# The first pair's normalisation in fewer sums, with a Newton root, and a changed order on GpSimd

## The chip, the cores and the metric

The kernel runs on one core of one Trainium2 chip. The metric is the device time of one execution in microseconds (us). Five engines run their own instruction streams and meet through semaphores: TensorE (PE in the rows; PEld is its weight load), VectorE (DVE), ScalarE (ACT), GpSimd (POOL) and SyncE (SP, which here only issues DMAs).

## The reference

Windowed attention, then two feed-forward layers on its output (2304 tokens of 512 values):

```python
scores = scale * q @ k.T                      # 4 x 8 heads, 576 tokens, 64 values a head
mask = (rel >= 0) & (rel < 64)                # each query sees the 64 keys up to its own
attn = exp(scores - max) / (sum + 1e-9)
x = (attn @ v), heads joined                  # 2304 x 512
rms = sqrt(mean(x * x, axis=-1) + 1e-6)
xn = x / rms * rms_g
y = (silu(xn @ w_gate) * (xn @ w_val)) @ w_out     # 512 -> 1536 -> 512
out = relu(y @ w_in) ** 2 @ w_down                 # 512 -> 2048 -> 512
```

## The kernel before, in words

Everything is written out by hand: five streams of instructions, one for each engine, in an order that the code fixes, and semaphores between them. No scheduler moves anything.

**Attention** (the first 80 us or so). The 144 query blocks of two heads each are taken in 18 groups of 8 blocks. For group g:

- PE (`slot(g)`) makes the scores of group g, then the product with v of group g-3, then transposes the probabilities of group g-2. Two score buffers alternate.
- DVE merges the two halves of each block's scores (L1468, COPY_PREDICATED), takes the negative maximum (L1475), inverts the row sums of group g-1 (L1480), and writes the masked transpose of group g-2 from PSUM into `probsT` (L1488).
- POOL adds 1e-9 to the row sums of group g-1 (L628), multiplies the negative maxima of group g by the scale (L632, `peak`), and multiplies the probabilities of group g-1 by the inverted sums (L635).
- ACT makes the exponentials of group g with the scaled maximum as bias (L1159), and copies finished attention output into `acts`.

Between these, work for what follows is placed at chosen groups: the split of the first two units' weights in a high and a low part (`high1_plain`, `low1_plain`, `high2_plain`, `low2_plain` on POOL), and the **first pair's normalisation**. A pair is 768 tokens (two halves of 384), and there are three. Its squares are made on POOL and ACT, PE sums them over the 512 values by products with a column of ones (`first_sums`, L817), DVE scales the sum (`mean_square`, L1420), ACT takes the root (`root`, L1119), DVE inverts it (`inverse`, L1425), POOL makes diagonals of the result (`diagonals`, L591), PE spreads them over all partitions (`spread_half`, L825), and DVE multiplies (`normalise`, L1428). ACT then rounds and DVE subtracts, which gives the two halves of a split operand (L1145, and `x_low`, L1460).

**Feed-forward layers** (the rest). PE multiplies split operands in three matmuls each (L844 to L846). The up projections run in units `u`, each of seven products p1 to p7 of six matmuls (a Strassen form). Unit u has POOL sum weights (`weight_sum`, L572 to L584) and multiply results (`h_a`, `h_b`, L672 and L683), DVE write three sums `ga`, `va`, `vb` (L1650, L1658, L1670) and low parts (`low1`, `low2`). The second and third pair's normalisation is made inside the units of the run before: `mean_square` in the unit with s == 8, `root` and `inverse` after it, `diagonals` on POOL at s == 9. PE holds these waits that the prediction speaks of:

```python
def p7(u, r):
    x_ready(u, r, "T3")
    if u > S0[r]:
        pe.wait_ge(c21_done, steps_done(u - 1))   # set by va of the unit before

if g == 18:
    pe.wait_ge(x_split, split_count(0, "B21"))    # set by x_low(0, "B21")
```

Of the kernel before, what the change touches and what calls it, by code (L numbers as in the profile page):

```python
# [29 lines left out]
BF16 = mybir.dt.bfloat16  # L30
ALU = mybir.AluOpType
# [3 lines left out]
P = 128  # L35
# [29 lines left out]
WARM = 6  # L65

# [90 lines left out]
def build(nc, qT, kT, v_rows, w_gate, w_val, w_out, gains, w_in, w_down, outT):  # L157
    with ExitStack() as ctx:
# [45 lines left out]
        rms = sb("rms", [P, TB], F32)  # L204
        assert top[0] <= nc.sbuf_usable_end, (top[0], nc.sbuf_usable_end)
# [4 lines left out]
        squares = [[sb(f"sq{n}_{k}", [P, PW], F32, at + k * PW * 4) for k in range(KT)]  # L210
                   for n, at in enumerate((hs_at, h_at + C1 * PW * 4))]
# [59 lines left out]
        sq_pool = sem("sq_pool")  # L271
        sq_done, sq_sum, ms_mm, ms_done = sem("sq_done"), sem("sq_sum"), sem("ms_mm"), sem("ms_done")
        rms_done, rinv_done, diag_done = sem("rms_done"), sem("rinv_done"), sem("diag_done")
# [134 lines left out]
        def _(sp):  # L408
# [128 lines left out]
        def _(pool):  # L537
# [48 lines left out]

            def diagonals(q):

                pool.wait_ge(rinv_done, q + 1)
                pool.wait_ge(ms_mm, q + 1)  # L590
                nc.gpsimd.tensor_tensor(diag[min(q, 1)][:].rearrange("p (n c) -> p n c", n=TB),  # L591
                                        ident[:].unsqueeze(1).broadcast_to([P, TB, P]),
                                        rms[:].unsqueeze(2).broadcast_to([P, TB, P]), ALU.mult).then_inc(diag_done, 1)
# [25 lines left out]
            def square_half(k, c):  # L619
                of = half_cols(0, k, c)  # L620
                nc.gpsimd.tensor_tensor(squares[0][k][:, c * NT:(c + 1) * NT], of, of, ALU.mult).then_inc(sq_pool, 1)

            for g in range(TAIL):
                n = g - N_LAG
                if 0 <= n < GROUPS:
                    total = sums[:, n % PR, :]
                    pool.wait_ge(exp_done, n + 1)
                    nc.gpsimd.tensor_scalar(total, total, 1e-9, None, ALU.add).then_inc(summed, 1)  # L628
                if g < GROUPS:
                    peak = neg_max[:, g % PR, :]  # L630
                    pool.wait_ge(maxed, g + 1)
                    nc.gpsimd.tensor_scalar(peak, peak, SCALE, None, ALU.mult).then_inc(biased, 1)  # L632
                if 0 <= n < GROUPS:
# [3 lines left out]
                if g == 5:  # L637
                    high1_plain(0)
                if g == 6:
                    low1_plain(0)  # L640
                if g == 7:
                    high2_plain(0)
                    low2_plain(0)
                if g in (8, 9):
                    pool.wait_ge(o_out, O_DONE[A_GROUP + 1])
                    for k in (2 * (g - 8), 2 * (g - 8) + 1):
                        square_half(k, 0)
                if g == 10:
                    high1_plain(1)
                    high2_plain(1)  # L650
                if g == 11:
                    pool.wait_ge(o_out, O_DONE[B_GROUP + 1])
                    square_half(0, 1)
                    square_half(1, 1)
                if g == 13:
                    diagonals(0)
                if g == 14:
                    low1_plain(1)
                if g == 15:
                    low2_plain(1)  # L660
# [69 lines left out]
        def _(pe):  # L730
# [82 lines left out]
            def first_sums(c, ps):  # L813

                for n in range(c * TB // 2, (c + 1) * TB // 2):
                    for k in range(KT):
                        mm = pe.matmul(ps[:, n:n + 1], squares[0][k][:, n * P:(n + 1) * P], ones[:, 0:1],  # L817
                                       start=k == 0, stop=k == KT - 1)
                if c == 1:
                    mm.then_inc(ms_mm, 1)  # L820
# [7 lines left out]
            def spread(q, banks):  # L828

                pe.wait_ge(diag_done, q + 1)  # L830
                for n in range(TB):
                    mm = spread_part(q, banks[n * P // NT], n)
                mm.then_inc(rb_mm, 1)

            def spread_half(c, ps):

                pe.wait_ge(diag_done, 1)
# [24 lines left out]
            for g in range(TAIL):  # L862
                slot(g)
                if g == 10:
# [221 lines left out]
        def _(act):  # L1086
# [22 lines left out]
            def square_half(k, c):  # L1109
                cols = slice(c * NT, (c + 1) * NT)  # L1110
                nc.scalar.activation(squares[0][k][:, cols], half_cols(0, k, c), ACT.Square).then_inc(sq_done, 1)
# [4 lines left out]
            def root(q):  # L1116

                act.wait_ge(ms_done, q + 1)
                nc.scalar.activation(rms[:], rms[:], ACT.Sqrt).then_inc(rms_done, 1)  # L1119
# [27 lines left out]
            for g in range(TAIL):  # L1147
# [15 lines left out]
                if g == B_GROUP + O_LAG:  # L1163
                    act.wait_ge(o_out, O_DONE[B_GROUP + 1])
                    square_half(2, 1)
                    square_half(3, 1)
                if g == 12:
                    root(0)
# [116 lines left out]
            for r in range(RUNS):  # L1285
                X, Y, Z = u_banks(r)[0:2], u_banks(r)[2], u_banks(r)[3]
                for u in range(S0[r], U0[r + 1]):
# [30 lines left out]
                    if r + 1 < PAIRS:  # L1318
# [8 lines left out]
                        if s == 8:  # L1327
                            root(r + 1)
# [67 lines left out]
        def _(dve):  # L1396
# [25 lines left out]
            def inverse(q):  # L1422

                dve.wait_ge(rms_done, q + 1)
                nc.vector.reciprocal(rms[:], rms[:]).then_inc(rinv_done, 1)  # L1425
# [37 lines left out]
            for g in range(TAIL):  # L1463
# [29 lines left out]
                if g == 12:  # L1493
                    mean_square(0, bank[5])
                if g == 13:
                    inverse(0)
# [55 lines left out]
            def square_sum(q, k):  # L1552
                dve.wait_ge(sq_done, 2 + KT * (q - 1) + k + 1)
# [73 lines left out]
            for r in range(RUNS):  # L1627
                X, Y, Z = u_banks(r)[0:2], u_banks(r)[2], u_banks(r)[3]
                for u in range(S0[r], U0[r + 1]):
# [14 lines left out]
                    if s == 9 and r + 1 < PAIRS:  # L1644
                        inverse(r + 1)
# [167 lines left out]
```

## Time and profile before

| | |
|---|---|
| median of 3 runs | 878.12 us (876.03 to 879.7) |
| the profiled execution | 876.42 us, its span 874.7 us |
| busy | PE 98%, DVE 68%, ACT 55%, POOL 53% of the span |
| granted TensorE clock | 0.998 of full speed in the mean |

The span is the time from the first to the last instruction of the profiled execution; what lies around it is 1.7 us. Busy shares are means over the whole span. Times in rows are us from the start of the span; "[x <-ENGINE tile]" is how long the engine stood idle before the row and what ended it.

### The profile page before, as it was taken

The numbers are of one execution on the slowest core, as the hardware profiler recorded it, in microseconds if no ns is written. First come the engines' busy times: TensorE is split into PE (matmuls) and PEld (weight loads), VectorE is DVE, ScalarE is ACT, GpSimd is POOL, SyncE is SP. The second block draws the span as 40 slices with busy tenths as digits, with TensorE's granted clock in tenths as the row PEclk, the third lists the DMA queues.
The fourth block names the chain that finished last, engine by engine and source line by source line (L and its number), as shares of the span: only waits on it lengthen the run. The fifth ranks groups of instructions, "written<-read, shape, count | busy, mean of one in ns | idle before, by whom it ended". The sixth has DMA issues, their size and how long they took to land.

```text
span 874.7 us, 16801 instructions
## 1 busy us (share of the span) xinstructions
PE 854.7 (98%) x6388; PEld 841.5 (96%) x6388; DVE 591.4 (68%) x728; ACT 478.8 (55%) x1005; POOL 466.0 (53%) x473
## 2 busy tenths in 40 slices
PE   7798999999999999999999999999999999999998
PEld 5687999999999999999999999999999999999998
DVE  4758675558567548755557767687577787577982
ACT  5887665545565645455555455454555454555451
POOL 3756398683589765388857368400187400386100
PEclk9999999999999999999999999999999999999999
DMA  8863122222222212222212222256632166522687
GB/s 281 263 220 87 49 73 73 61 61 61 84 73 70 70 55 61 79 73 73 73 55 64 81 67 73 56 158 228 218 87 72 56 218 184 176 73 97 182 256 237
DMA packets 107871, 100.18 MB, mean 115 GB/s; under 512 B 6928, under 2 KB 85776, under 8 KB 107792
## 3 DMA queue, kind: packets, MB, share of 16 engines
q1 hardware_dynamic: 92544, 84.14, 32.3%
q10 hardware_dynamic: 15248, 14.98, 4.9%
q8 instruction: 51, 0.84, 0.4%
q14 instruction: 28, 0.23, 0.1%
HBM read 79.69 MB, written 19.40 MB: 113 GB/s over the span
## 4 chain that ended last, share of the span: by engine, by line
PE 90%; DVE 5%; issue 2%; ACT 1%; DMA 1%; POOL 1%; DVEq 0%; ACTq 0%; POOLq 0%
PE banks L844 29%; PE banks L845 28%; PE banks L846 28%; PE banks L803 1%; PE banks L745 1%; DVE probsT L1488 1%; ACT probs L1159 1%; PE banks L817 1%; DMA w_kept<-stash 1%; PE banks L777 1%; DVE acts L1428 0%; DVE banks L1468 0%; DVE d_lo L1574 0%; DVE xc_lo L1460 0%; PE banks L753 0%
## 5 line engine op out<-in xcount | busy, mean ns | idle before, releaser
L844 PE MATMUL banks<-xc_hi,w_hi 128*128 128x384 f32 x844 | 282.6, 335 | 0.2 <-DVE xc_lo L1460 0.2
L846 PE MATMUL banks<-xc_hi,w_lo 128*128 128x384 f32 x844 | 281.9, 334 | 0.0
L845 PE MATMUL banks<-xc_lo,w_hi 128*128 128x384 f32 x844 | 281.9, 334 | 0.0
L844 PE MATMUL banks<-hs_hi,d_hi 128*128 128x384 f32 x544 | 182.4, 335 | 2.3 <-DVE d_lo L1574 2.2
L846 PE MATMUL banks<-hs_hi,d_lo 128*128 128x384 f32 x544 | 181.8, 334 | 0.0
L845 PE MATMUL banks<-hs_lo,d_hi 128*128 128x384 f32 x544 | 181.7, 334 | 0.0
L844 PEld LDWEIGHTS banks<-xc_hi,w_hi 128*128 128x128 f32 x844 | 158.4, 188 | 0.6 <-DVE xc_lo L1460 0.4
L845 PEld LDWEIGHTS banks<-xc_lo,w_hi 128*128 128x128 f32 x844 | 158.4, 188 | 0.0
L846 PEld LDWEIGHTS banks<-xc_hi,w_lo 128*128 128x128 f32 x844 | 158.4, 188 | 0.0
L1405 DVE TENSOR_TENSOR w_lo<-w_raw,w_hi 128x1024 fp32r<-128x1024 f32 x58 | 77.1, 1329 | 81.8 <-ACT w_hi L1090 81.8
L572 POOL TENSOR_TENSOR w_raw<-w_raw 128x256 f32<-128x256 f32 x58 | 60.8, 1047 | 134.0 <-DMA w_raw<-in_w_in 113.6
L1566 DVE TENSOR_TENSOR hs_lo<-h,hs_hi 128x768 fp32r<-128x768 f32 x68 | 68.6, 1009 | 80.5 <-ACT hs_hi L1090 80.2
L1090 ACT ACTIVATE hs_hi<-h 128x768 fp32r<-128x768 f32 x68 | 57.4, 844 | 104.4 <-PE banks L846 99.9
L1090 ACT ACTIVATE w_hi<-w_raw 128x1024 fp32r<-128x1024 f32 x116 | 109.3, 942 | 0.0
L844 PEld LDWEIGHTS banks<-hs_hi,d_hi 128*128 128x128 f32 x544 | 102.1, 188 | 4.0 <-DVE d_lo L1574 2.9
L845 PEld LDWEIGHTS banks<-hs_lo,d_hi 128*128 128x128 f32 x544 | 102.1, 188 | 0.0
L846 PEld LDWEIGHTS banks<-hs_hi,d_lo 128*128 128x128 f32 x544 | 102.1, 188 | 0.0
L690 POOL TENSOR_TENSOR d_lo<-d_raw,d_hi 128x512 fp32r<-128x512 f32 x36 | 54.9, 1524 | 68.2 <-ACT d_hi L1090 68.2
L683 POOL TENSOR_TENSOR h<-sbb,vb 128x384 f32<-128x384 f32 x34 | 55.7, 1638 | 26.1 <-ACT sbb L1199 25.9
L1414 DVE TENSOR_TENSOR w_lo<-w_raw,w_hi 128x768 fp32r<-128x768 f32 x58 | 69.4, 1197 | 0.0
L1205 ACT ACTIVATE sa<-ga 128x384 f32<-128x384 f32 x58 | 30.5, 526 | 67.3 <-DVE ga L1650 67.1
L1090 ACT ACTIVATE c_t<-banks 128x384 f32<-128x384 f32 x58 | 28.5, 492 | 65.3 <-PE banks L846 65.3
(114 smaller groups left out, 1342.5 us busy)
## 6 DMA issues: line engine op xcount, KB each, us to landing
w_kept<-stash SPq DMA_DIRECT2D x56, 256.0 KB, 3.1
w_raw<-in_w_gate SPq DMA_DIRECT2D x36, 256.0 KB, 2.9
w_raw<-in_w_val SPq DMA_DIRECT2D x72, 128.0 KB, 2.8
d_raw<-in_w_out SPq DMA_DIRECT2D x36, 256.0 KB, 2.6
d_raw<-in_w_down SPq DMA_DIRECT2D x32, 256.0 KB, 3.0
v_sb<-in_v_rows SPq DMA_DIRECT2D x16, 384.0 KB, 5.0
w_raw<-in_w_in SPq DMA_DIRECT2D x24, 256.0 KB, 2.7
w_raw<-in_w_in SPq DMA_DIRECT2D x48, 128.0 KB, 2.6
```

What stands on the lines that cost most here:

```text
L572: nc.gpsimd.tensor_tensor(raw_part(u, RAW_S3), raw_part(u, RAW_A11), raw_part(u, RAW_A21), ALU.subtract).then_inc(s_add, 1)
L683: nc.gpsimd.tensor_tensor(h_half(n, 1), sbuf_b[:], vb[:], ALU.mult).then_inc(hb_done, 1)
L690: nc.gpsimd.tensor_tensor(d_lo[m % 2][:], d_raw[m % 2][:], d_hi[m % 2][:].bitcast(F32), ALU.subtract).then_inc(dlo_done, 1)
L745: mm = pe.matmul(to, q_sb[par][r, b * WIN:(b + 1) * WIN], both, start=b > 0, stop=True)
L844: pe.matmul(ps, w_h, v_h, start=first, stop=False, skip_group_check=joined)
L845: pe.matmul(ps, w_h, v_l, start=False, stop=False, skip_group_check=joined)
L846: return pe.matmul(ps, w_l, v_h, start=False, stop=last, skip_group_check=joined)
L1090: nc.scalar.activation(to, of, ACT.Copy).then_inc(done, 1)
L1205: nc.scalar.activation(sa[:], ga[:], ACT.Silu if first_layer(r) else ACT.Relu).then_inc(act_a_done, 1)
L1405: nc.vector.tensor_tensor(w_lo[u % 2][:, to], w_raw[u % 2][:, of], w_hi[u % 2][:, to].bitcast(F32), ALU.subtract).then_inc(lo1_done, 1)
L1414: nc.vector.tensor_tensor(w_lo[u % 2][:, to], w_raw[u % 2][:, of], w_hi[u % 2][:, to].bitcast(F32), ALU.subtract).then_inc(lo2_done, 1)
L1566: nc.vector.tensor_tensor(hs_lo[m % 2][:], h_chunk(r, chunk_of(r, m - M0[r])), hs_hi[m % 2][:].bitcast(F32), ALU.subtract).then_inc(hlo_do ...
```

## The change

Its parts, in the order of the diff:

- The first and second `load_w` are issued at i = 4 and 6 of SP's load loop, not 1 and 3; the first two `load_d` at 10 and 11, not 9 and 10.
- The first pair's squares go two blocks at a time (`square_two`, one POOL instruction for 128x768 where there were two of 128x384), the two halves of the 512 values are added (on POOL for the first half of the tokens, on DVE for the second), and `first_sums` takes 12 matmuls for each half of the tokens where it took 24. It stands after slots 11 and 13, not 10 and 12.
- `root` on ACT and `inverse` on DVE are gone. `inverse_root` on DVE makes the inverse root of all three pairs from an integer seed and two Newton steps: seven instructions on 128x6 values, each waiting for the one before.
- The first pair's diagonals are made in two halves, at groups 13 and 14.
- POOL scales the maximum of group g before it adds to the sums of group g-1, where the order was the other way.
- The split of the first weights moves on POOL from groups 5 to 7, 10, 14 and 15 to groups 12 and 14 to 18.

```diff
-                if i in (1, 3):
-                    load_w((i - 1) // 2)
-                if i in (9, 10):
-                    load_d(i - 9)
+                if i in (4, 6):
+                    load_w((i - 4) // 2)
+                if i in (10, 11):
+                    load_d(i - 10)
...
+            def first_diagonals(c):
+                n = TB // 2
+                pool.wait_ge(rinv_done, STEPS)
...
             for g in range(TAIL):
                 n = g - N_LAG
-                if 0 <= n < GROUPS:
-                    total = sums[:, n % PR, :]
-                    pool.wait_ge(exp_done, n + 1)
-                    nc.gpsimd.tensor_scalar(total, total, 1e-9, None, ALU.add).then_inc(summed, 1)
                 if g < GROUPS:
                     peak = neg_max[:, g % PR, :]
                     pool.wait_ge(maxed, g + 1)
                     nc.gpsimd.tensor_scalar(peak, peak, SCALE, None, ALU.mult).then_inc(biased, 1)
                 if 0 <= n < GROUPS:
+                    total = sums[:, n % PR, :]
+                    pool.wait_ge(exp_done, n + 1)
+                    nc.gpsimd.tensor_scalar(total, total, 1e-9, None, ALU.add).then_inc(summed, 1)
...
+                if g in (8, 9):
+                    pool.wait_ge(o_out, O_DONE[A_GROUP + 1])
+                    square_two(g - 8, 0)
+                if g == 10:
+                    pool.wait_ge(sq_pool, 2)
+                    nc.gpsimd.tensor_tensor(sq_all[:, 0:2, 0:NT], sq_all[:, 0:2, 0:NT], sq_all[:, 2:4, 0:NT],
+                                            ALU.add).then_inc(sq_added, 1)
+                if g == 11:
+                    pool.wait_ge(o_out, O_DONE[B_GROUP + 1])
+                    square_two(0, 1)
+                if g == 12:
                     high1_plain(0)
-                if g == 6:
+                if g == 13:
+                    first_diagonals(0)
+                if g == 14:
+                    first_diagonals(1)
                     low1_plain(0)
...
-                if g == 14:
+                if g == 17:
                     low1_plain(1)
...
-                if g == 10:
+                if g == 11:
                     pe.wait_ge(consts, CONSTS)
-                    pe.wait_ge(sq_pool, KT)
+                    pe.wait_ge(sq_added, 1)
                     first_sums(0, bank[5])
-                if g == 12:
-                    pe.wait_ge(sq_pool, KT + 2)
-                    pe.wait_ge(sq_done, 2)
+                if g == 13:
+                    pe.wait_ge(sq_added, 2)
                     first_sums(1, bank[5])
...
+            def inverse_root(q):
+                done = STEPS * q
+                dve.wait_ge(ms_done, q + 1)
+                nc.vector.tensor_scalar(guess[:].bitcast(I32), rms[:].bitcast(I32), -0.5, ROOT_SEED, ALU.mult,
+                                        ALU.add).then_inc(rinv_done, 1)
+                for n, (by, plus) in enumerate(ROOT_STEPS):
+                    dve.wait_ge(rinv_done, done + 1 + 3 * n)
+                    nc.vector.tensor_tensor(resid[:], guess[:], guess[:], ALU.mult).then_inc(rinv_done, 1)
+                    dve.wait_ge(rinv_done, done + 2 + 3 * n)
+                    nc.vector.scalar_tensor_tensor(out=resid[:], in0=resid[:], scalar=by, in1=rms[:], op0=ALU.mult,
+                                                   op1=ALU.mult).then_inc(rinv_done, 1)
+                    dve.wait_ge(rinv_done, done + 3 + 3 * n)
+                    nc.vector.scalar_tensor_tensor(out=guess[:], in0=resid[:], scalar=plus, in1=guess[:], op0=ALU.add,
+                                                   op1=ALU.mult).then_inc(rinv_done, 1)
...
                 if g == 12:
+                    dve.wait_ge(sq_pool, 3)
+                    dve.wait_ge(sq_done, 1)
+                    nc.vector.tensor_tensor(sq_all[:, 0:2, NT:PW], sq_all[:, 0:2, NT:PW], sq_all[:, 2:4, NT:PW],
+                                            ALU.add).then_inc(sq_added, 1)
+                if g == 13:
                     mean_square(0, bank[5])
-                if g == 13:
-                    inverse(0)
+                    inverse_root(0)
...
                     if s == 9 and r + 1 < PAIRS:
-                        inverse(r + 1)
+                        inverse_root(r + 1)
```

How POOL's stream stands at groups 16 and 17, the last two with a maximum. Before:

```order
L628 TENSOR_SCALAR sums<-sums 128x8
L632 TENSOR_SCALAR neg_max<-neg_max 128x8
L635 TENSOR_TENSOR probs_114<-probs_114,sums 128x512
L628 TENSOR_SCALAR sums<-sums 128x8
L632 TENSOR_SCALAR neg_max<-neg_max 128x8
L635 TENSOR_TENSOR probs_111<-probs_111,sums 128x512
```

And now:

```order
L646 TENSOR_SCALAR neg_max<-neg_max 128x8
L650 TENSOR_SCALAR sums<-sums 128x8
L652 TENSOR_TENSOR probs_113<-probs_113,sums 128x512
L629 CAST w_hi_56<-w_raw_60 128x768
L633 CAST w_hi_56<-w_raw_60 128x256
L646 TENSOR_SCALAR neg_max<-neg_max 128x8
L650 TENSOR_SCALAR sums<-sums 128x8
L652 TENSOR_TENSOR probs_110<-probs_110,sums 128x512
L618 TENSOR_TENSOR w_lo_58<-w_raw_60,w_hi_56 128x768
```

The maximum now stands ahead of the sums in each group, and the low part of the second unit's weights (L618) follows right behind the probabilities of the last group with a maximum.

DVE's stream at the unit with s == 9 of the first run, where the second pair's root is inverted. Before:

```order
L1405 TENSOR_TENSOR w_lo_57<-w_raw_59,w_hi_55 128x1024
L1425 RECIPROCAL rms<-rms 128x6
L1650 TENSOR_TENSOR ga<-banks,c_t 128x384
L1658 TENSOR_TENSOR va<-banks,c_u 128x384
```

And now:

```order
L1410 TENSOR_TENSOR w_lo_57<-w_raw_59,w_hi_55 128x1024
L1431 TENSOR_SCALAR guess<-rms 128x6
L1435 TENSOR_TENSOR resid<-guess 128x6
L1437 SCALAR_TENSOR_TENSOR resid<-resid,rms 128x6
L1440 SCALAR_TENSOR_TENSOR guess<-resid,guess 128x6
L1435 TENSOR_TENSOR resid<-guess 128x6
L1437 SCALAR_TENSOR_TENSOR resid<-resid,rms 128x6
L1440 SCALAR_TENSOR_TENSOR guess<-resid,guess 128x6
L1670 TENSOR_TENSOR ga<-banks,c_t 128x384
```

Seven small instructions stand where one stood, between the low part of the weights and `ga`.

## Rows read from the trace of the kernel before

**Rows 1.** Waits of PE from 80 us on: who for whom, us, times, longest

```profile
PE banks L844 <- DVE d_lo L1574: 2.2, 2, 1.1
```

**Rows 2.** Chain that ended last, 0 to 100 us, its longest "issue": start, us, what

```profile
28.04 1.67 issue
```

**Rows 3.** Timeline of DVE in the attention: start, us, line, tiles

```profile
41.03 0.20 DVE L1480 RECIPROCAL sums<-sums 128x8 f32<-128x8 f32 x1
41.16 1.19 DVE L1488 TENSOR_TENSOR probsT<-banks,mask_t 128x1024 f32<-128x1024 f32 x1
...
45.05 1.23 DVE L1488 TENSOR_TENSOR probsT<-banks,mask_t 128x1024 f32<-128x1024 f32 x1 [0.55 <-PE banks L777]
...
51.42 1.23 DVE L1488 TENSOR_TENSOR probsT<-banks,mask_t 128x1024 f32<-128x1024 f32 x1 [1.07 <-PE banks L777]
52.86 0.69 DVE L1468 COPY_PREDICATED banks<-pick,banks 128x512 f32<-128x512 uint16 x1 [0.22 <-PE banks L745]
53.66 0.69 DVE L1475 TENSOR_REDUCE neg_max<-banks 128x8 f32<-128x512 f32 x1
54.27 0.19 DVE L1480 RECIPROCAL sums<-sums 128x8 f32<-128x8 f32 x1
...
58.27 0.69 DVE L1468 COPY_PREDICATED banks<-pick,banks 128x512 f32<-128x512 uint16 x1 [0.91 <-PE banks L745]
...
64.12 1.18 DVE L1488 TENSOR_TENSOR probsT<-banks,mask_t 128x1024 f32<-128x1024 f32 x1
65.22 1.13 DVE L1428 SCALAR_TENSOR_TENSOR acts<-acts,gain,banks 128x384 f32<-128x384 f32 x2
...
76.03 1.17 DVE L1488 TENSOR_TENSOR probsT<-banks,mask_t 128x1024 f32<-128x1024 f32 x1
...
78.17 0.95 DVE L1460 TENSOR_TENSOR xc_lo<-acts,xc_hi 128x768 fp32r<-128x768 f32 x1
...
81.34 1.49 DVE L1447 TENSOR_TENSOR sq<-acts 128x768 f32<-128x768 f32 x1
```

**Rows 4.** Timeline of POOL in the attention

```profile
40.76 0.24 POOL L628 TENSOR_SCALAR sums<-sums 128x8 f32<-128x8 f32 x1
41.08 0.24 POOL L632 TENSOR_SCALAR neg_max<-neg_max 128x8 f32<-128x8 f32 x1
...
54.44 0.24 POOL L632 TENSOR_SCALAR neg_max<-neg_max 128x8 f32<-128x8 f32 x1 [0.73 <-DVE neg_max L1475]
54.64 1.06 POOL L635 TENSOR_TENSOR probs<-probs,sums 128x512 f32<-128x512 f32 x1
...
65.31 1.82 POOL L601 TENSOR_TENSOR w_lo<-w_raw,w_hi 128x768 fp32r<-128x768 f32 x1
...
81.97 1.44 POOL L576 TENSOR_TENSOR w_raw<-w_raw 128x256 f32<-128x256 f32 x1
```

**Rows 5.** Timeline of PE at the second sums and at the first split product

```profile
54.34 2.81 PE L817 MATMUL banks<-ones,sq 128*128 128x1 f32 x24
...
79.17 0.44 PE L844 MATMUL banks<-xc_hi,w_hi 128*128 128x384 f32 x1 [0.18 <-DVE xc_lo L1460]
```

**Rows 6.** Timeline of DVE at s == 8 and 9 of the first run

```profile
145.60 1.23 DVE L1405 TENSOR_TENSOR w_lo<-w_raw,w_hi 128x1024 fp32r<-128x1024 f32 x1 [3.09 <-ACT w_hi L1090]
...
152.88 1.23 DVE L1405 TENSOR_TENSOR w_lo<-w_raw,w_hi 128x1024 fp32r<-128x1024 f32 x1 [2.04 <-ACT w_hi L1090]
154.02 0.18 DVE L1425 RECIPROCAL rms<-rms 128x6 f32<-128x6 f32 x1
...
155.56 0.56 DVE L1658 TENSOR_TENSOR va<-banks,c_u 128x384 f32<-128x384 f32 x1 [0.48 <-PE banks L846]
```

**Rows 7.** Timeline of POOL one unit earlier, and PE's first matmul of p7

```profile
146.02 1.68 POOL L683 TENSOR_TENSOR h<-sbb,vb 128x384 f32<-128x384 f32 x1 [1.94 <-ACT sbb L1199]
...
149.28 0.74 POOL L584 TENSOR_TENSOR w_raw<-w_raw 128x256 f32<-128x256 f32 x1
...
157.44 0.33 PE L844 MATMUL banks<-xc_hi,w_hi 128*128 128x384 f32 x1
```

More of the change, by code:

```diff
@@ L30 @@
 BF16 = mybir.dt.bfloat16
+I32 = mybir.dt.int32
 ALU = mybir.AluOpType
@@ L65 @@
 WARM = 6
+ROOT_SEED = float(0x5F1FFFF9)
+ROOT_STEPS = ((-0.703952253, 0.703952253 * 2.38924456), (-0.5, 1.5))
+STEPS = 1 + 3 * len(ROOT_STEPS)
 def last_group(seq):
@@ L204, in build @@
         rms = sb("rms", [P, TB], F32)
+        guess = sb("guess", [P, TB], F32)
+        resid = sb("resid", [P, TB], F32)
         assert top[0] <= nc.sbuf_usable_end, (top[0], nc.sbuf_usable_end)
         T1, T2, T3, T4 = [sb(f"T{n + 1}", [P, PW], F32, temp_at + n * PW * 4) for n in range(4)]
-        squares = [[sb(f"sq{n}_{k}", [P, PW], F32, at + k * PW * 4) for k in range(KT)]
-                   for n, at in enumerate((hs_at, h_at + C1 * PW * 4))]
+        sq_all = sb("sq_all", [P, KT, PW], F32, hs_at)
+        squares = [[sq_all[:, k, :] for k in range(KT)],
+                   [sb(f"sq{k}", [P, PW], F32, h_at + (C1 + k) * PW * 4) for k in range(KT)]]
         diag = [sq[0] for sq in squares]
@@ L585, in weight_sum @@
                                             ALU.subtract).then_inc(s_add, 1)
+            def first_diagonals(c):
+                n = TB // 2
+                pool.wait_ge(rinv_done, STEPS)
+                pool.wait_ge(ms_mm, 1)
+                nc.gpsimd.tensor_tensor(diag[0][:, c * NT:(c + 1) * NT].rearrange("p (n c) -> p n c", n=n),
+                                        ident[:].unsqueeze(1).broadcast_to([P, n, P]),
+                                        guess[:, c * n:(c + 1) * n].unsqueeze(2).broadcast_to([P, n, P]),
+                                        ALU.mult).then_inc(diag_done, 1)
             def diagonals(q):
[L589 removed]
+                pool.wait_ge(rinv_done, STEPS * (q + 1))
                 pool.wait_ge(ms_mm, q + 1)
[L591 removed]
+                nc.gpsimd.tensor_tensor(diag[1][:].rearrange("p (n c) -> p n c", n=TB),
                                         ident[:].unsqueeze(1).broadcast_to([P, TB, P]),
[L593 removed]
+                                        guess[:].unsqueeze(2).broadcast_to([P, TB, P]), ALU.mult).then_inc(diag_done, 1)
             def by_unit(of):
@@ L617, in high2_plain, with square_two @@
                                       raw_part(u, RAW_A22)).then_inc(hi2_done, 1)
-            def square_half(k, c):
-                of = half_cols(0, k, c)
-                nc.gpsimd.tensor_tensor(squares[0][k][:, c * NT:(c + 1) * NT], of, of, ALU.mult).then_inc(sq_pool, 1)
+            def square_two(kh, c):
+                of = x_block(0, kh, c)
+                nc.gpsimd.tensor_tensor(sq_all[:, 2 * kh:2 * kh + 2, c * NT:(c + 1) * NT], of, of,
+                                        ALU.mult).then_inc(sq_pool, 1)
             for g in range(TAIL):
                 n = g - N_LAG
-                if 0 <= n < GROUPS:
-                    total = sums[:, n % PR, :]
-                    pool.wait_ge(exp_done, n + 1)
-                    nc.gpsimd.tensor_scalar(total, total, 1e-9, None, ALU.add).then_inc(summed, 1)
                 if g < GROUPS:
@@ L636, in _ @@
                                             by_unit(sums[:, n % PR, :]), ALU.mult).then_inc(scaled, 1)
-                if g == 5:
+                if g in (8, 9):
[9 more added lines that the diff above has]
+                if g == 12:
                     high1_plain(0)
-                if g == 6:
+                if g == 13:
+                    first_diagonals(0)
+                if g == 14:
+                    first_diagonals(1)
                     low1_plain(0)
-                if g == 7:
+                if g == 15:
                     high2_plain(0)
                     low2_plain(0)
[L644 to L647, printed above, removed]
-                if g == 10:
+                if g == 16:
                     high1_plain(1)
                     high2_plain(1)
[L651 to L654, printed above, removed]
-                if g == 13:
-                    diagonals(0)
-                if g == 14:
+                if g == 17:
                     low1_plain(1)
-                if g == 15:
+                if g == 18:
                     low2_plain(1)
@@ L815, in first_sums @@
                 for n in range(c * TB // 2, (c + 1) * TB // 2):
-                    for k in range(KT):
+                    for k in range(2):
                         mm = pe.matmul(ps[:, n:n + 1], squares[0][k][:, n * P:(n + 1) * P], ones[:, 0:1],
-                                       start=k == 0, stop=k == KT - 1)
+                                       start=k == 0, stop=k == 1)
                 if c == 1:
@@ L1164, in _ @@
                     act.wait_ge(o_out, O_DONE[B_GROUP + 1])
[L1165 to L1168, printed above, removed]
+                    nc.scalar.activation(sq_all[:, 2:4, NT:PW], x_block(0, 1, 1), ACT.Square).then_inc(sq_done, 1)
                 if g in (15, 16):
```

23 lines of the change are left out of this document (5 added, 18 removed).

## Prediction

> **What bounds the kernel now.** I read the waits of PE first. From 80 us to the end it waits in one place worth naming, 2.2 us for DVE's low part of w_out [rows 1], which the change does not touch; the rest is matmul behind matmul. So the time is the moment at which PE's unbroken work begins, plus what is put between its matmuls later. That moment is 79.17 us, when the first product that needs `x_low(0, "B21")` starts, right behind that instruction on DVE (78.17, 0.95 long) [rows 3, 5]. Ahead of it lie 18 groups of attention, and the timelines of DVE, POOL and PE tell what sets their pace.
>
> I mark a group by the start of `probsT` on DVE, X(n) for group n: X(7) = 41.16, X(8) = 45.05, X(9) = 51.42, X(12) = 64.12, X(15) = 76.03 [rows 3]. On the chain there are waits of PE without a releaser ("issue"), the longest 1.67 us at 28.04 [rows 2]. I take them for instructions that come late.
>
> **Maximum first.** It takes POOL's 0.32 us for the sums (40.76 to 41.08 [rows 4]) out of ACT's way to the next exponential. But DVE inverts the sums of group g-1 between the maximum of g and X(g-2), in order, and POOL now adds to the sums only after it has scaled that maximum. DVE's own loop becomes: X to its next instruction 1.10 (64.12 to 65.22), merge to maximum 0.80 (52.86 to 53.66), maximum to its scaling on POOL 0.78 (53.66 to 54.44), scaling to sums 0.32, sums to reciprocal 0.27 (40.76 to 41.03), reciprocal to X 0.13 (41.03 to 41.16): 3.4 us a group [rows 3, 4]. Before, the reciprocal stood 0.61 behind the maximum (53.66 to 54.27 [rows 3]) if the sums were ready; now 1.37. That is 0.76 us of idle DVE in each group. Where PE is late anyway it is hidden; where DVE sets the pace it counts in full.
>
> **Start to X(8).** Stepping the loop through the timeline, X(0) comes 0.76 late, the wait at 28.04 swallows what has gathered, and the groups behind it pay again, less what PE's lateness covers: X(8) at 45.2, 0.2 us later than before, if instructions arrive as they did. The move of the weights takes 1 MB from ahead of 24 us and puts it behind 26 us, next to the longest wait. Bounds: without any such wait X(8) = 15.9 + 8 x 3.4 = 43.1 (a gain of 1.9); if the longest doubles, 1.5 worse.
>
> **X(8) to X(12)**, before 19.07 us, which holds PE's 24 sums twice, and the root on ACT with a table load on each side of it. Now: four loops, 13.6. The first sums follow X(8) by 2.9 us (51.42 to 54.34), take half of 2.8, 1.4, and the merge of group 12 starts 1.2 behind them (57.1 to 58.27): 5.5 behind X(8), where the loop has 3.4 + 1.1 = 4.5 [rows 3, 5]: 1.0. DVE's addition of squares is as large as x_low, 0.95 [rows 3]. The second sums lie beside DVE's work. The scaling and seven Newton instructions on 128x6 values: I give each the 0.16 to 0.2 of a reciprocal of that size (0.18 at 154.02 [rows 6]). The step from one instruction to one that needs it is its length plus about 0.1 (merge 0.69, step 0.80 [rows 3]), so 0.27; seven steps and an exit: 2.0. Together 17.6, a gain of 1.5. The dependent step is the unknown: 0.2 to 0.4 makes 0.5 less to 0.9 more.
>
> **X(12) to the first split product.** Before, 15.05 us, DVE back to back. Now 0.76 for each of three groups, and 0.1 once for POOL with a diagonal and `low1_plain(0)`: 2.4 lost. And one thing more. DVE's instruction with two SBUF operands at 81.34 took 1.49 us where x_low of the same size took 0.95, and POOL's weight sum at 81.97 took 1.44 where 0.74 is usual: they ran one after the other, each waiting for the other's end [rows 3, 4, 7]. Now `low1_plain(1)`, 1.82 long as at 65.31 [rows 4], follows the probabilities of group 16. Counting from POOL's sums: reciprocal 0.27, X(15) 0.4, probabilities from 0.56 to 1.6 (length 1.06 [rows 4]), `low1_plain(1)` to 3.4; x_low is due 2.14 behind X(15) (76.03 to 78.17 [rows 3]), at 2.53. It waits 0.9. So 3.3 lost. Attention in sum: +0.2 - 1.5 + 3.3 = 2.0 us later.
>
> The Trainium skill (SBUF — State Buffer, "SBUF: two separate sides") states the turn-taking as a rule: a VectorE instruction with two SBUF inputs and a GpSimd instruction that reads SBUF hold one port pair in turn, and the later one blocks in full. By that rule the trace agrees on instructions of this size, and the rule makes no exception for small ones, which bears on the next part.
>
> **The units at s == 9**, in runs 0 and 1. Taking the root from ACT gives nothing, since PE has no wait there. On DVE the reciprocal (154.02) becomes seven instructions ahead of `ga` and `va`. `va` starts at 155.56 and ends at 156.1; PE's p7 of the next unit waits for it and starts at 157.44 [rows 6, 7]: 1.3 us of cover. Undisturbed, 154.02 + 6 x 0.27 + 0.1 lets `ga` start at 155.8 and `va` end at 156.9: hidden, 0.5 left. But six of the seven have two SBUF operands, and POOL is busy. One unit earlier its h_b starts 0.4 behind DVE's low part (145.60) and is done 2.0 behind it, and three weight sums of 0.74 follow, the last from 149.28 [rows 6, 7]. Without the table load on ACT, h_b stands so in this unit too: 153.3 to 154.9, then the sums. In the gap of 0.1 between dependent instructions POOL's next takes its turn: the first product waits 0.6 for h_b, three more wait 0.75 each, 2.8 in all. `ga` then starts at 158.5, `va` ends at 159.5, and PE waits 2.0, in each of two units: 4.0 us. Bounds: 0 (small instructions are not held up) and 2 x 2.6 (the seed is blocked as well).
>
> **The sum.** 876.42 (the profiled execution) + 2.0 + 4.0 = 882.4. The median of the runs is 1.7 above that execution, so 884.1 against 878.12: 0.7% slower.
>
> **The rivals.** 0.5% of this kernel, 4.4 us, is about what its measurement can tell from no change.
>
> 1. *Small instructions pass POOL.* The units cost nothing, attention 2.0: 880.1. For it: no row shows a 128x6 instruction blocked. Against it: the larger ones alternate. It decides at 0.5 us of blocking.
> 2. *Instructions for PE arrive earlier*, with the weights gone from the first 24 us: X(8) at 43.1 and 882.2 with the units' waits. Against it: the longest wait gets a weight load beside it.
> 3. *They arrive later* in the same place: 1.5 to 3 more, 886 to 887.
> 4. *Maximum first pays (the other side).* If ACT's chain through POOL sets the groups, each of the first fifteen gains 0.3, the Newton part 1.5, and the units cost nothing: 872. It decides by whether DVE's idle before the reciprocal is covered; behind X(12) it is not, since DVE has no gap there.
> 5. *The Newton chain is no shorter than the root*: steps of 0.4 cost 0.9 in the attention and in each unit, of which 0.5 there is covered: 882 in the place of rival 1.
>
> **How the numbers follow.** My forecast has 0.46; rivals 1 and 5 have 0.24 and 0.06, rival 2 0.10, rival 3 0.06, rival 4 0.08. Slower by over 0.5% are the forecast and rival 3 but for 0.07: 0.45. Faster: rival 4, 0.08. The rest, 0.47, lies within. The range leaves out rival 4 and the far end of rival 3: 877.5 to 887.5; the forecast's own is 882 to 886.5.
>
> **What would show it.** X(8) near 45, X(12) near 62.8; 0.7 us of idle DVE before each reciprocal, put down to POOL's sums; PE's first split product behind x_low at 81.2, and that x_low longer than 0.95; at s == 9 of runs 0 and 1 seven DVE instructions over 4 us, and a PE wait of 2 us for `va`. If PE waits for nothing there, the second term is wrong; if X steps by 3.1, the first.

## The result, and the profile after

| | before | changed |
|---|---|---|
| median of the runs | 878.25 us (876.03 to 882.72, 16 runs) | 882.13 us (877.75 to 886.13, 16 runs) |
| ratio, 95% interval | | 1.0043, 1.0028 to 1.0058 |
| profiled execution, its span | 876.42 us, 874.7 us | 880.06 us, 878.3 us |

The change makes the kernel 0.43% slower. The profiled execution of the changed kernel is 3.6 us longer than that of before, and the rows of the two account for it. Every ratio below is against the kernel before on the same chip.

The group of the page that carries the feed-forward products, and the waits of PE from 80 us on (who for whom, us, times, longest), answer to [rows 1]:

```profile
L864 PE MATMUL banks<-xc_hi,w_hi 128*128 128x384 f32 x844 | 283.3, 336 | 2.1 <-DVE va L1678 1.9
```

```profile
PE banks L864 <- DVE d_lo L1594: 2.2, 2, 1.1
PE banks L864 <- DVE va L1678: 1.9, 2, 1.0
```

The second line is new: PE waits for `va` twice, 1.9 us in all, where before nothing above 0.3 us but the old wait for `d_lo` was left.

The waits of DVE in the attention (0 to 82 us) have a new head as well. Before, this line read 4.1 us in 7 times.

```profile
DVE sums L1496 <- POOL sums L650: 12.6, 17, 1.5
```

Timeline of DVE in the attention of the changed kernel, for [rows 3]:

```profile
43.70 1.23 DVE L1504 TENSOR_TENSOR probsT<-banks,mask_t 128x1024 f32<-128x1024 f32 x1
...
58.26 0.15 DVE L1425 TENSOR_SCALAR rms<-banks 128x6 f32<-128x6 f32 x1
58.45 0.17 DVE L1431 TENSOR_SCALAR guess<-rms 128x6 int32<-128x6 int32 x1
...
59.66 0.17 DVE L1440 SCALAR_TENSOR_TENSOR guess<-resid,guess 128x6 f32<-128x6 f32 x1
59.74 0.69 DVE L1484 COPY_PREDICATED banks<-pick,banks 128x512 f32<-128x512 uint16 x1
...
61.90 0.20 DVE L1496 RECIPROCAL sums<-sums 128x8 f32<-128x8 f32 x1 [0.68 <-POOL sums L650]
62.02 1.18 DVE L1504 TENSOR_TENSOR probsT<-banks,mask_t 128x1024 f32<-128x1024 f32 x1
...
76.24 1.18 DVE L1504 TENSOR_TENSOR probsT<-banks,mask_t 128x1024 f32<-128x1024 f32 x1
...
78.39 1.67 DVE L1476 TENSOR_TENSOR xc_lo<-acts,xc_hi 128x768 fp32r<-128x768 f32 x1
```

X(8) is at 43.70, X(12) at 62.02, X(15) at 76.24. The reader is to see three things: the seven Newton instructions follow each other every 0.20 us (58.45 to 59.66) and nothing disturbs them here; DVE idles 0.68 us before the reciprocal; and `x_low(0, "B21")` takes 1.67 us, not 0.95. POOL, and PE's next work, in the same stretch, for [rows 4, 5]:

```profile
77.42 1.83 POOL L618 TENSOR_TENSOR w_lo<-w_raw,w_hi 128x768 fp32r<-128x768 f32 x1
79.34 0.82 POOL L650 TENSOR_SCALAR sums<-sums 128x8 f32<-128x8 f32 x1
```

```profile
77.48 1.40 PE L823 MATMUL banks<-probsT,v_sb 64*64 64x64 f32 x60 [2.53 <-DVE probsT L1504]
...
80.12 0.69 PE L864 MATMUL banks<-xc_hi,w_hi 128*128 128x384 f32 x1 [0.20 <-DVE xc_lo L1476]
...
81.95 0.34 PE L864 MATMUL banks<-xc_hi,w_hi 128*128 128x384 f32 x1
```

The low part of the weights on POOL (77.42) ends at 79.25, and x_low gets through only then. PE's first split product behind that x_low ("the first split product" in what follows) starts at 80.12, 0.95 later than before. PE had been idle for 2.53 us ahead of 77.48, where the kernel before has 1.67 us ahead of 77.26, and behind that its clock fell. The stretches show it (engines, then granted clock, DMA share, GB/s):

```profile
77.00:78.00 1.00, 0.52 (x33) 0.52 (x37) 1.00 (x3) 1.00 (x8) 1.00 (x2) 1.00 0.00 0
78.00:79.00 1.00, 1.00 (x41) 0.88 (x34) 1.00 (x2) 0.76 (x3) 1.00 (x1) 0.60 0.00 0
...
80.00:81.00 1.00, 0.88 (x3) 0.89 (x4) 0.87 (x3) 0.63 (x1) 0.68 (x2) 0.50 0.35 94
```

The first six split products take 1.83 us (80.12 to 81.95) at the lower level, 1.2 GHz, for the most part; before they took 1.16 (79.17 to 80.33) at a granted clock of 1.00. Now the unit at s == 9 of the first run, DVE and then POOL, for [rows 6, 7]:

```profile
154.53 1.23 DVE L1410 TENSOR_TENSOR w_lo<-w_raw,w_hi 128x1024 fp32r<-128x1024 f32 x1 [2.04 <-ACT w_hi L1109]
155.67 0.98 DVE L1431 TENSOR_SCALAR guess<-rms 128x6 int32<-128x6 int32 x1
156.69 0.65 DVE L1435 TENSOR_TENSOR resid<-guess 128x6 f32<-128x6 f32 x1
157.38 0.17 DVE L1437 SCALAR_TENSOR_TENSOR resid<-resid,rms 128x6 f32<-128x6 f32 x1
157.57 0.59 DVE L1440 SCALAR_TENSOR_TENSOR guess<-resid,guess 128x6 f32<-128x6 f32 x1
158.20 0.17 DVE L1435 TENSOR_TENSOR resid<-guess 128x6 f32<-128x6 f32 x1
158.40 0.59 DVE L1437 SCALAR_TENSOR_TENSOR resid<-resid,rms 128x6 f32<-128x6 f32 x1
159.03 0.17 DVE L1440 SCALAR_TENSOR_TENSOR guess<-resid,guess 128x6 f32<-128x6 f32 x1
...
159.61 0.55 DVE L1678 TENSOR_TENSOR va<-banks,c_u 128x384 f32<-128x384 f32 x1
```

```profile
154.95 1.68 POOL L703 TENSOR_TENSOR h<-sbb,vb 128x384 f32<-128x384 f32 x1 [0.89 <-ACT sbb L1206]
156.58 0.73 POOL L583 TENSOR_TENSOR w_raw<-w_raw 128x256 f32<-128x256 f32 x1
157.40 0.75 POOL L587 TENSOR_TENSOR w_raw<-w_raw 128x256 f32<-128x256 f32 x1
158.22 0.75 POOL L591 TENSOR_TENSOR w_raw<-w_raw 128x256 f32<-128x256 f32 x1
```

The same seven instructions that took 0.17 each at 58 us now take 0.17 to 0.98. Each long one ends where a POOL instruction ends (the seed at 156.65 with POOL's `h` at 156.63; the second, 156.69 + 0.65 = 157.34, with POOL's 156.58 + 0.73 = 157.31). Behind the seed the next is held at once; behind each of the other long ones one DVE instruction gets in before POOL's next. From the seed's start to that of `ga`, directly behind the last of them, are 3.5 us. PE waits behind `va`:

```profile
160.21 0.44 PE L864 MATMUL banks<-xc_hi,w_hi 128*128 128x384 f32 x1 [0.95 <-DVE va L1678]
```

So the 3.6 us are: 0.95 at the first split product, 0.7 of a fallen clock right behind it (the low part at s == 9 stands at 154.53 against 152.88, 1.65 later), and 0.95 in each of two units.

### The profile page after: what moved, and what is told of

Same layout as the page of the kernel before. It is cut to its first block, busy times and chain, and to the rows that moved or that the text cites. A ratio compares the mean times of both kernels' runs of the same rounds, so it can differ in the third digit from the quotient of the medians.

```text
span 878.3 us, 16762 instructions
## 1 busy us (share of the span) xinstructions
PE 852.2 (97%) x6364; PEld 838.3 (95%) x6364; DVE 600.1 (68%) x747; ACT 470.4 (54%) x995; POOL 470.6 (54%) x472
## 4 chain that ended last, share of the span: by engine, by line
PE 87%; DVE 8%; issue 2%; POOL 1%; ACT 1%; DVEq 0%; ACTq 0%; POOLq 0%
PE banks L864 28%; PE banks L866 28%; PE banks L865 28%; DVE probsT L1504 2%; DVE neg_max L1491 1%; PE banks L823 1%; DVE banks L1484 1%; ACT probs L1169 1%; PE banks L765 1%; DVE xc_lo L1476 0%; DVE d_lo L1594 0%; DVE acts L1444 0%; POOL neg_max L646 0%; POOL sums L650 0%; PE banks L773 0%
```

## The experiments

They ask three things: whether the two losses that the rows show (maximum first, Newton ahead of `ga` and `va`) are losses of the measured time, whether the turns with POOL are what makes the short instructions long, and whether the collision at x_low, the fallen clock and the later weight loads cost time.

### The Newton steps in the units

**Alone in the kernel before.** Only the units' root is replaced by the seven instructions, at s == 9; the first pair and all orders stay.

```
     # DVE, s == 9
-    inverse(r + 1)
+    inverse_root(r + 1)
     # ACT, s == 8
-    root(r + 1)
```

> The kernel before with one edit: the second and third pair's inverse root by the seven DVE instructions at s == 9, in the place of the square root on ACT and the reciprocal; the first pair and the attention as before. My theory: PE waits 0.9 to 1.0 us for va in each of two units, span 1.9 us longer with the same attention, ratio 1.0020 to 1.0025. Rival (the two table loads saved on ACT give something back): no wait, ratio 1.000 or less.

Median 880.65 us, ratio 1.0030 (1.0019 to 1.0040). DVE at s == 9, then PE's waits:

```profile
156.34 0.98 DVE L1435 TENSOR_SCALAR guess<-rms 128x6 int32<-128x6 int32 x1
157.35 0.65 DVE L1439 TENSOR_TENSOR resid<-guess 128x6 f32<-128x6 f32 x1
```

```profile
PE banks L850 <- DVE va L1678: 1.9, 2, 1.0
```

The seven take 0.98, 0.65, 0.17, 0.59, 0.17, 0.59 and 0.17 us: pattern and wait are those of the changed kernel, so they come from this edit and from nothing else in it. The waits are 1.9 us; the ratio, 2.6 us with an interval of 1.7 to 3.5, holds them. The expected ratio was lower, and the profiled span is 4.3 us longer, not 1.9: X(12) came at 66.42 in this execution, 2.3 us later than before, though the attention is unchanged.

**The root back on ACT.** In the changed kernel the second and third pair take their root on ACT and a reciprocal on DVE, as before.

```
     # ACT
+    if s == 8:
+        root(r + 1)
     # DVE, s == 9
-    inverse_root(r + 1)
+    nc.vector.reciprocal(guess[:], rms[:])
```

> The changed kernel, but the second and third pair's root as before (square root on ACT, one reciprocal on DVE); the first pair keeps the Newton steps. My theory (seven DVE instructions ahead of va in the units with s == 9 make PE wait 1.0 us in each): both waits for va gone, the attention as in the changed kernel, span 876.3, ratio 1.0020 to 1.0025. Rival (the waits are taken up by slack later): span 878, ratio 1.004.

Median 880.37 us, ratio 1.0033 (1.0018 to 1.0047). The waits for `va` are gone. In its place stand 1.3 us for the DMA of `w_kept`, in three waits, and in this execution X(12) comes at 64.03. The ratio lies 0.0010 under the changed kernel's, inside both intervals, and is above what was expected: this run alone proves no gain.

**Newton behind `vb`.** The same seven instructions, but behind `ga`, `va`, `vb` and the low part.

```
-    if s == 9 and r + 1 < PAIRS:
-        inverse_root(r + 1)        # ahead of ga, va, vb
     ...
     low2(u + 1)
+    if s == 9 and r + 1 < PAIRS:
+        inverse_root(r + 1)
```

> The changed kernel with the units' seven Newton instructions moved on DVE behind vb and low2 of the same unit, where DVE stands idle for 2 us. My theory: no wait of PE for va, diagonals still in time for the spread one unit later, span 876.3, ratio 1.0020 to 1.0025, as with the root on ACT. Rival (the chain is a cost wherever it stands, since it delays the next low part, w_lo): a wait of PE for w_lo or x_low in the next unit, span 877 to 878.

Median 879.72 us, ratio 1.0020 (1.0007 to 1.0033). PE waits for nothing of `va`. The chain stands in a free stretch of POOL and runs at its own pace:

```profile
161.00 0.16 DVE L1431 TENSOR_SCALAR guess<-rms 128x6 int32<-128x6 int32 x1
...
162.19 0.17 DVE L1440 SCALAR_TENSOR_TENSOR guess<-resid,guess 128x6 f32<-128x6 f32 x1
```

POOL's `diagonals` start at 162.44, three microseconds later than in the changed kernel (159.27), and PE has no wait for them: nothing needed the Newton result early. Span (877.0) and ratio came out near what was expected.

**One operand in PSUM.** Same place, same count, but the mean square and the intermediate stay in PSUM, so that no instruction of the chain reads two SBUF operands.

```
-    nc.vector.tensor_tensor(resid[:], guess[:], guess[:], ALU.mult)
+    nc.vector.tensor_tensor(y, m, guess[:], ALU.mult)       # y, m: columns of the PSUM bank
     (and the two scalar_tensor_tensor: y in the place of resid, guess in that of rms)
```

> The changed kernel with the units' mean square and the Newton intermediate held in PSUM, so that none of the seven instructions has two SBUF operands; same number, same place, same chain. Theory of turns with POOL at the SBUF port: the instructions that took 0.59 to 0.98 us fall to 0.17 to 0.25, the chain from 3.5 us to 1.6, no wait of PE for va, span 876.3, ratio 1.002. Rival (small dependent DVE instructions are slow there for another reason, semaphores or a busy queue): lengths and waits stay, span 878.

Median 880.36 us, ratio 1.0028 (1.0014 to 1.0043). DVE and POOL at s == 9:

```profile
157.87 0.16 DVE L1434 TENSOR_SCALAR guess<-banks 128x6 int32<-128x6 int32 x1
...
158.27 0.17 DVE L1440 SCALAR_TENSOR_TENSOR banks<-banks,guess 128x6 f32<-128x6 f32 x1
...
159.09 0.17 DVE L1443 SCALAR_TENSOR_TENSOR guess<-banks,guess 128x6 f32<-128x6 f32 x1
```

```profile
157.16 1.67 POOL L703 TENSOR_TENSOR h<-sbb,vb 128x384 f32<-128x384 f32 x1 [0.90 <-ACT sbb L1206]
158.79 0.73 POOL L583 TENSOR_TENSOR w_raw<-w_raw 128x256 f32<-128x256 f32 x1
```

This is the run that settles the mechanism. The chain lies on POOL's `h` and weight sum as in the changed kernel, and every instruction takes 0.16 or 0.17 us where 0.98, 0.65 and 0.59 stood. What blocked them was the reading of SBUF beside POOL, not the dependence between them, and not the length of the chain. The chain of 1.3 us is covered, and the wait for `va` is gone. What that is worth in time this run doesn't show: its ratio lies above the expected 1.002, its interval overlaps the changed kernel's, and X(12) came at 64.94.

### Maximum first

**Alone in the kernel before.**

```
 for g in range(TAIL):            # POOL
+    if g < GROUPS:               # scale the maximum of g
+        ...
     if 0 <= n < GROUPS:          # 1e-9 to the sums of g-1
         ...
-    if g < GROUPS:
-        ...
```

> The kernel before with one edit: POOL scales the maximum of group g before it adds to the sums of group g-1. My theory: DVE idle 0.7 us before every reciprocal, X steps of at least 3.4, behind X(12) 0.7 lost in each of three groups, partly hidden by PE's waits ahead of X(8): first split product 1.5 to 3 us later than 79.17, span 876.5 to 878, ratio 1.0015 to 1.0035. Rival (ACT's exponentials set the groups, and get 0.3 us each): first split product earlier than 79, ratio 0.998 or less.

Median 881.17 us, ratio 1.0036 (1.0023 to 1.0050). DVE's waits, 0 to 80 us, and a row of its timeline:

```profile
DVE sums L1479 <- POOL sums L632: 12.9, 17, 1.4
```

```profile
67.55 0.20 DVE L1479 RECIPROCAL sums<-sums 128x8 f32<-128x8 f32 x1 [0.68 <-POOL sums L632]
```

X(12) is at 63.24 and X(15) at 77.39: 14.15 us for three groups, against 11.91 before [rows 3], so 0.75 a group. The swap is a loss by itself. In the one profiled execution the groups ahead of X(12) hide it (X(12) is even 0.9 earlier than before); the three behind it don't. PE's idle time ahead of `slot(18)` is 2.51 us here as well, and the clock fell to 0.50 behind it. That execution took 878.25 us, 2.9 less than the median, so its rows show only a part of the 0.36%, which is just above the expected range; the first split product came at 81.30, 2.1 us later than before.

**Taken out of the changed kernel** (sums first again, the rest as changed).

> The changed kernel with POOL's order of before (sums of group g-1, then the maximum of group g). My theory (DVE's loop goes through POOL: 0.68 us of idle before each reciprocal): X steps of 3.1 to 3.3 where PE and the instruction waits allow, the three groups behind X(12) 0.7 shorter each, PE's first split product at 77 to 78 us and not 80.12, no 2.5 us gap of PE ahead of it and no fall of the clock behind it; span 874.5 to 875.5 (from 878.3), ratio to before 1.000 to 1.002. Rival (maximum first shortens ACT's chain and pays, the loss is elsewhere): the exponentials start later, the first split product at 80 or behind, ratio 1.004 or more.

Median 878.81 us, ratio 1.0018 (1.0006 to 1.0030), 0.0025 under the changed kernel. It keeps 1.9 us of waits for `va`. But X(12) at 63.30 and X(15) at 75.92 are 12.6 us apart, not 11.9, since POOL's place behind X(12) now holds a diagonal and `low1_plain(0)`: the first of the three steps is 4.36 and not 3.66, the other two are as before. x_low still takes 1.78. So the first split product came at 79.90, not at the expected 77 to 78, and against the expectation the clock fell to 0.50 here too, behind an idle time of 1.63 us.

### The collision at x_low, and the clock behind it

**`low1_plain(1)` one group later.**

```
-    if g == 17:
-        low1_plain(1)
     if g == 18:
+        low1_plain(1)
         low2_plain(1)
```

> The changed kernel with low1_plain(1) on POOL one group later, behind the probabilities of group 17, so that no POOL instruction stands beside x_low(0, B21). My theory (turns at the SBUF port): that x_low falls from 1.67 to 0.95 us, PE's first split product starts 0.7 us earlier against X(15) (3.2 us behind it, not 3.9), ratio 1.003 to 1.004 (from 1.0043). Rival (low1_plain(1) now stands in the way of x_low(B12) and of the first weight sums, and PE waits for those): the first product is earlier, but a new wait of PE before 100 us takes it back, ratio 1.0043 or more.

Median 881.89 us, ratio 1.0050 (1.0031 to 1.0068). The DVE timeline shows the collision gone:

```profile
79.37 1.18 DVE L1503 TENSOR_TENSOR probsT<-banks,mask_t 128x1024 f32<-128x1024 f32 x1
...
81.51 0.97 DVE L1475 TENSOR_TENSOR xc_lo<-acts,xc_hi 128x768 fp32r<-128x768 f32 x1
...
84.49 2.59 DVE L1462 TENSOR_TENSOR sq_all<-acts 128x768 f32<-128x768 f32 x1
```

x_low is back from 1.67 to 0.97, and meets no weight part. The addition of squares behind it pays instead (2.59 where 1.49 stood), off PE's path. From X(15) to the first split product are 3.17 us (79.37 to 82.54), 3.88 in the changed kernel. The time didn't follow: the ratio is not under the changed kernel's, and 1.003 to 1.004 was expected. Its profiled execution came to X(12) at 65.16, 3.1 us later than the changed one's, which hides 0.7, and the clock fell to 0.50 behind `slot(18)` here too.

**Twelve products in PE's gap.** Ahead of `slot(18)` PE multiplies the identity by itself twelve times into a free bank; the result is unused. (The profile has 24 records of them, L885.)

> The changed kernel with 12 matmuls on the identity into an unused bank ahead of slot 18, where PE stands idle 2.5 us; their result is used by nothing. Theory of the clock (PE's idle time from 75 us is what its clock falls after, at 78.5 to 81.7, and the first split products take 0.7 us longer for it): granted clock 1.00 from 75 to 90 us, the same start of the first split product, unbroken work 0.7 us earlier, ratio 1.003 to 1.0035. Rival (the fall comes of something else): the clock falls as before, or more; ratio 1.0043 or above.

Median 881.27 us, ratio 1.0042 (1.0030 to 1.0055). PE's timeline:

```profile
76.00 2.84 PE L885 MATMUL banks<-ident 128*128 128x128 f32 x24
78.77 1.15 PE L823 MATMUL banks<-probsT,v_sb 64*64 64x64 f32 x60
...
81.33 0.44 PE L864 MATMUL banks<-xc_hi,w_hi 128*128 128x384 f32 x1 [0.82 <-DVE xc_lo L1479]
...
82.48 0.33 PE L864 MATMUL banks<-xc_hi,w_hi 128*128 128x384 f32 x1
```

The clock stays at 1.00 and six split products take 1.15 us, 0.7 less than in the changed kernel's profile. The time is the same, where 1.003 to 1.0035 was expected. The run is inconclusive: the clock was also 1.00 in this stretch of the run with PSUM operands, which fills nothing, so the fall doesn't come in every execution, and a single profile can't say how much the median carries.

### The weight loads

**Earlier again**, at the sequences of before, in the changed kernel.

```
-    if i in (4, 6):
-        load_w((i - 4) // 2)
-    if i in (10, 11):
-        load_d(i - 10)
+    if i in (1, 3):
+        load_w((i - 1) // 2)
+    if i in (9, 10):
+        load_d(i - 9)
```

> The changed kernel with the first two weight loads and the first two w_out loads at the places of before (i = 1 and 3, 9 and 10). My forecast had the instruction waits of PE moved rather than removed by this part, at a price of 0.2 us to X(8) with bounds of -1.9 and +1.5. If the move is worth nothing: ratio 1.0035 to 1.005, as the changed kernel. If late weights help (rival, loads ahead of 24 us delay instructions): X(8) later than 45, ratio 1.005 to 1.006. If they hurt (loads beside the longest wait): ratio 1.0025 to 1.0035.

Median 881.87 us, ratio 1.0051 (1.0038 to 1.0064), not separable from 1.0043 and at the bound between what was expected if the move is worth nothing (up to 1.005) and if late weights help (from 1.005). Its profiled execution has the long PE wait back, in the chain that ended last:

```profile
29.78 1.76 issue
```

X(8) is at 48.55. The late loads thus cost nothing measurable, and whether they gain is open: the ratios can't tell 0.0008, X(8) lies between 43.70 and 46.10 in the profiled executions of the changed kernel and of those variants above that keep its loads, and waits of this kind of 1.45 and 1.81 us occur with late loads too (at 48.11 and 31.79 in the next kernel).

### Both losses out

**Sums first and Newton behind `vb`** in the changed kernel; half sums, Newton root for the first pair, split diagonals, late loads and late weight parts stay.

> The changed kernel with two edits: sums first on POOL, and the units' Newton chain behind vb and low2; the loads and the split of the first weights stay where the change put them. If the two losses add (1.0043 to 1.0018 and to 1.0020 one at a time): ratio 0.9995. If so, what is left to the kernel with everything mended (0.998) is 1.3 us for the places of loads and weight splits, of which the trace should show 0.7 us at x_low(B21) behind low1_plain(1) and 0.7 us at group 15, whose maximum waits on POOL for a diagonal and low1_plain(0). Rival (the gains do not add, since instruction waits take up the slack): ratio 1.001 to 1.002.

Median 876.03 us, ratio 0.9974 (0.9961 to 0.9987), lower than the 0.9995 expected.

**The same, with loads and POOL's weight parts where they stood before.**

> The changed kernel with what my theory holds for the losses taken out: sums first on POOL, the weight loads and the split of the first weights at the groups of before (12, 15 and 16 for the second unit), the units' Newton chain behind vb and low2. Kept: half of the token sums, the Newton steps, the diagonals in halves. My theory: X(12) some 1.5 us ahead of 64.12, nothing lost behind it, no PE wait for va, first split product at 77.5 to 78, span 873 to 873.5, ratio 0.998 to 0.999, the fastest of all. Rival (instruction waits and the clock's falls in the first 60 us give back what the shorter work gains): first product at 79 or later, ratio 1.000 to 1.002.

Median 876.23 us, ratio 0.9980 (0.9965 to 0.9994). DVE and PE of the latter:

```profile
74.66 1.17 DVE L1506 TENSOR_TENSOR probsT<-banks,mask_t 128x1024 f32<-128x1024 f32 x1
...
76.79 0.95 DVE L1478 TENSOR_TENSOR xc_lo<-acts,xc_hi 128x768 fp32r<-128x768 f32 x1
```

```profile
77.80 0.45 PE L866 MATMUL banks<-xc_hi,w_hi 128*128 128x384 f32 x1 [0.18 <-DVE xc_lo L1478]
```

X(12) is at 62.77, x_low takes 0.95 again, and the first split product starts at 77.80, 1.4 us earlier than before. The former still pays for x_low (`78.48`, 1.77 long) and is as fast by its median. Its profiled execution (877.03) is one of its longer ones, with the first split product at 80.31, so for it the gain is seen in the runs' times alone. Both beat the two kernels: what is left of the change is a gain of some 0.2%, and the swap on POOL and the place of the units' Newton steps turned it into a loss. Which of the parts left brings the gain (half sums, Newton steps in the place of the root on ACT, split diagonals) no run takes apart. The pieces add up: alone they cost 0.36% and 0.30%, the rest gains 0.26%, in sum 0.40% against the 0.43% measured. Taken out of the changed kernel one at a time they give back 0.25% and 0.23%, together 0.69%; the difference of 0.21% lies within the intervals of the four ratios.

## Why the prediction was right or wrong

Forecast 884.1 with 877.5 to 887.5; the median was 882.13. Direction, range and the two mechanisms held; the size was 6.0 us forecast, 3.9 measured between the medians. Against the profiled executions, where the sum was made, it was 6.0 against 3.6. That the attention came near its forecast (+0.95, or +1.65 with the clock, for +2.0) is luck in part: two of its terms missed in opposite directions. Step by step:

- **Maximum first, 0.76 us of idle DVE a group: right.** Rows with 0.68 to 0.87 us from X(8) on, put down to POOL's sums, 12.6 us in all; 0.75 a group with the swap alone. That it is hidden where PE is late and counts behind X(12) held in those traces. Rival 4 falls.
- **Start to X(8), +0.2: measured -1.35, wrong by 1.55.** X(8) came at 43.70 for 45.2, since the wait of 1.67 us at 28.04 that the sum kept did not come: the longest of that kind in the changed kernel's chain is 1.18 us, at 45.89, behind X(8). That is rival 2 in this execution. It is not settled as a gain of the moved loads, as the other kernels' X(8) shows.
- **X(8) to X(12), -1.5: measured -0.75.** The interval is 18.32 us, 17.6 forecast, 19.07 before. The Newton part was cheaper than forecast (1.48 us from 58.26 to the merge at 59.74, not 2.0; the step is 0.20, not 0.27, so the low end of the bounds). The late instructions, gone from before X(8), appear here: 0.86 and 1.13 us of DVE waiting for PE behind that 1.18.
- **X(12) to the first split product, +3.3: measured +3.05.** 18.10 against 15.05 us. x_low was held 0.72 us by `low1_plain(1)`, 0.9 forecast, and the run that moved that instruction gave it back. Attention in sum +0.95 for +2.0.
- **The units, +4.0: measured +1.9. This is the step that failed, in size and not in kind.** The forecast let `h_b` hold the first product for 0.6 and three weight sums hold one instruction each for 0.75, 2.8 us of blocking, with steps of 0.27; so it had the end of `va` 3.4 late and PE 2.0. The runs showed the same four POOL instructions in the way, but 2.1 us of blocking. `h_b` held the seed (0.98 for 0.17, which the forecast had only as a bound). Each weight sum held one instruction for 0.42 to 0.48 beyond its own length (0.65, 0.59, 0.59 for 0.17), not for 0.75. The held instruction starts 0.11, 0.17 and 0.18 us behind the sum (156.69 against 156.58, 157.57 against 157.40, 158.40 against 158.22) and ends with it. And the undisturbed step is 0.20. The chain is 3.5 us long where 4.5 was forecast, and with the same cover of 1.3 us PE waits 1.0, not 2.0. Rival 1, that small instructions pass, fell with both kernels that have the chain ahead of `ga`. The Trainium skill (SBUF — State Buffer, "SBUF: two separate sides") states the turns for a VectorE instruction with two SBUF inputs or in one of its two-port performance modes, beside a GpSimd instruction. By that rule the trace agrees for small instructions with two SBUF inputs: 0.59 to 0.65 us beside POOL and 0.17 with one operand in PSUM. Whether the seed, with its one operand, was held (0.98) because of such a mode, no run here shows.
- **Not in the sum: the clock.** PE's idle time of 2.5 us ahead of 77.48, a consequence of the stretched groups (1.67 before, 2.51 with the swap alone), was followed by a clock down to 0.50, and the slower products cost 0.7 us in the profiled execution. How much of the median it is stays open.
- **The offset** of 1.7 between profile and median was 2.1 for the changed kernel. Its profiled execution reached X(12) earlier (62.02) than those of its variants with maximum first (63.24 to 66.86), which fits; what decides from execution to execution how late PE's instructions come in the first 60 us was not tried.

## What to carry to other kernels

A short chain of tiny VectorE instructions is not priced by its lengths but by what GpSimd does beside it: put it where GpSimd is idle or behind the work that TensorE waits for, or keep one operand in PSUM. In a loop over several engines, moving a 0.3 us instruction out of one engine's way puts it, and the wait for its inputs, in another's; ask which of the two has no slack. And an edit made of parts is worth taking apart: here two of its parts hid a gain of the rest.

## What the runs showed of the hardware

- DVE instructions on 128x6 values with two SBUF operands took 0.17 us alone and 0.59 to 0.65 when held by one of POOL's back-to-back instructions, while every second one passed at 0.17; an int32 `tensor_scalar` with a single SBUF operand took 0.98 beside POOL's `h` and 0.16 to 0.17 without POOL work, which the forecast had only as a bound. With one operand in PSUM (the seed: its only one), all took 0.16 to 0.17 beside the same POOL work.
- It goes both ways: POOL's addition to 128x8 sums, one SBUF operand, took 0.82 us at 79.34 while x_low ran to 80.06, where 0.24 is usual [rows 4].
- Two dependent DVE instructions of that size start 0.20 us apart, for a length of 0.17, in SBUF and in PSUM.
- The granted clock fell to 0.50 behind an idle time of PE of 2.5 us ahead of `slot(18)` in six of the seven profiled executions that leave it unfilled, and behind one of 1.6 to 1.7 us in one of five.
